# A Strassen-like MLP kernel: C11, C22 and x^T stored ahead of other transfers, and four instruction queues reordered

## What is computed

```python
kv  = einsum('bhsd,bhse->bhde', k, v)            # 8 batches, 8 heads, 576 rows, 64 columns
out = einsum('bhsd,bhde->bhse', q, kv)
x   = out / sqrt(mean(out*out, -1) + 1e-6) * g_norm   # -> 4608 tokens x 512
# first layer (d_ff = 1536)
x = (sigmoid(x @ w_gate) * (x @ w_val)) @ w_out
# second layer
g = x @ w2_gate
out = (g * sigmoid(g) * (x @ w2_val)) @ w2_out    # 4608 x 512, float32
```

## Time and profile before

| | |
|---|---|
| median of three runs | 1748.85 us |
| profiled execution, its own time | 1745.59 us |
| its span (first to last instruction) | 1743.8 us |
| TensorE busy | 1720.7 us, 99% |
| VectorE busy | 1206.9 us, 69% |
| ScalarE busy | 888.8 us, 51% |
| GpSimd busy | 377.8 us, 22% |
| mean granted share of TensorE's clock | 0.997 |
| moved by DMA | 366.93 MB, 210 GB/s |

### The profile page before, as it was taken

One profiled execution on the slowest core, in us unless ns is written; L12 is line 12 of the kernel. 1 busy time (PEld: TensorE's weight loads), 2 busy tenths in 40 slices (PEclk: granted clock), 3 DMA queues, 4 the chain that ended last, 5 costly groups with the idle time before them and its releaser, 6 DMA issues.

```text
span 1743.8 us, 30846 instructions
## 1 busy us (share of the span) xinstructions
PE 1720.7 (99%) x11190; PEld 1689.6 (97%) x11190; DVE 1206.9 (69%) x1938; ACT 888.8 (51%) x1709; POOL 377.8 (22%) x326
## 2 busy tenths in 40 slices
PE   9999999999999999999999999999999999999998
PEld 7899899999999999999998999999999999999998
DVE  4977677787666678666679877787666668655556
ACT  5766566655444445444456555555444445444444
POOL 5722222013111125111136000013111125111111
PEclk9999999999999999999999999999999999999999
DMA  9787786586555576555655555566555567555553
GB/s 243 252 286 196 262 255 200 213 302 224 199 200 199 200 243 228 200 199 200 212 163 215 195 199 200 198 245 240 202 196 202 196 221 239 167 176 190 184 185 92
DMA packets 200151, 366.93 MB, mean 210 GB/s; under 512 B 49984, under 2 KB 160064, under 8 KB 200000
## 3 DMA queue, kind: packets, MB, share of 16 engines
q1 hardware_dynamic: 199776, 364.56, 62.4%
q10 hardware_dynamic: 224, 0.39, 0.1%
HBM read 234.36 MB, written 130.55 MB: 209 GB/s over the span
## 4 chain that ended last, share of the span: by engine, by line
PE 83%; POOL 1%; DVE 1%; DMA 1%; issue 1%; SPq 0%; ACT 0%; DVEq 0%; ACTq 0%; POOLq 0%
PE ps L841 81%; PE ps L764 1%; PE ps L698 0%; DMA wops<-in_q_dram 0%; POOL arena L1659 0%; PE ps L683 0%; DVE arena L1407 0%; DMA xraw<-x 0%; PE ps L688 0%; DVE arena L1389 0%; PE ps L782 0%; PE ps L710 0%; SPq L415 0%; POOL wops L1604 0%; POOL wops L1603 0%
## 5 line engine op out<-in xcount | busy, mean ns | idle before, releaser
L841 PE MATMUL ps<-xo,wa 128*128 128x384 f32 x6048 | 1078.9, 336 | 5.9 <-ACT arena L1038 3.2
L841 PEld LDWEIGHTS ps<-xo,wa 128*128 128x128 f32 x6048 | 1048.6, 188 | 9.6 <-issue 3.6
L1038 ACT ACTIVATE arena<-ps 128x384 f32<-128x384 f32 x648 | 317.1, 491 | 576.9 <-PE ps L841 575.2
L1389 DVE TENSOR_TENSOR arena<-ps,arena 128x384 f32<-128x384 f32 x648 | 352.6, 553 | 362.5 <-PE ps L841 284.3
L841 PE MATMUL ps<-hop,wb 128*128 128x384 f32 x3024 | 538.1, 335 | 1.1 <-DVE arena L1407 0.9
L841 PEld LDWEIGHTS ps<-hop,wb 128*128 128x128 f32 x3024 | 523.0, 188 | 5.0 <-issue 1.7
L1659 POOL TENSOR_TENSOR arena<-arena 128x384 f32<-128x384 f32 x144 | 147.5, 1049 | 734.1 <-DVE arena L1389 734.1
L1339 DVE TENSOR_TENSOR hop<-arena,hop 128x384 fp32r<-128x384 f32 (+1 forms) x396 | 275.9, 719 | 32.8 <-ACT hop L1020 26.8
L1020 ACT ACTIVATE hop<-arena 128x384 fp32r<-128x384 f32 (+1 forms) x396 | 233.4, 609 | 63.6 <-DVE arena L1407 36.0
L1052 ACT ACTIVATE arena<-arena 128x384 f32<-128x384 f32 x216 | 112.7, 522 | 65.2 <-DVE arena L1389 65.1
L1407 DVE TENSOR_TENSOR arena<-arena 128x384 f32<-128x384 f32 x216 | 127.9, 594 | 20.3 <-DVE arena L1389 1.4
(11 more groups left out here) (75 smaller groups left out, 781.9 us busy)
## 6 DMA issues: line engine op xcount, KB each, us to landing
xo<-x_operands SPq DMA_DIRECT2D x168, 768.0 KB, 6.2
x_operands<-xo SPq DMA_DIRECT2D x84, 768.0 KB, 5.3
x<-arena SPq DMA_DIRECT2D x120, 384.0 KB, 3.2
arena<-x SPq DMA_DIRECT2D x96, 384.0 KB, 4.6
xraw<-x SPq DMA_DIRECT2D x22, 768.0 KB, 6.1
wops<-in_moe_w_gate_dram SPq DMA_DIRECT2D x24, 256.0 KB, 4.8
wops<-in_moe_w_val_dram SPq DMA_DIRECT2D x24, 256.0 KB, 4.6
wops<-in_moe_w_out_dram SPq DMA_DIRECT2D x48, 128.0 KB, 2.3
```

The costliest lines, as they stand in the source:

```text
L841: mm = pe.matmul(dst, lhsT, rhs, start=(pr in (1, 5, 2) and c == 0 and i == 0), stop=(c == 1 and i == 2), skip_group_check=(pr in (6, 7, 4 ...
L1038: nc.scalar.activation(dst, X(side), ACT.Copy).then_inc(copied, 1)
L1389: nc.vector.tensor_tensor(dst, acc, buf, ALU.add).then_inc(summed, 1)
```

## The change

Nothing is computed differently, and no instruction of an engine is added or taken away. Instructions move in four queues; TensorE's and GpSimd's own order stay as they are.

- SyncE, at the end of each block: the stores of C11 and C22 go ahead of the third and fourth x operand of the next block. The store of the unit's x^T goes ahead of the stores of C21 and C12. In the blocks of the very first pass the load of the rows of the unit after next also goes ahead of C21 and C12; it stood at the start of the next block.
- ScalarE: in window 1 the copy of a unit's x^T goes ahead of the split of x operand 1 of the next block; in window 2 it goes ahead of the split of operand 7. In a pass's first block the SUMMED split of the fourth set goes behind the copy of product 7, side 0. In block 18 it goes further, behind the copy of side 1.
- VectorE: in block 18 the SUMMED split of set 21 goes behind the hidden values of C11 and C22. In block 17 the two sums that take C21 from its banks (`total_21`) go ahead of the split of operand 5 and of S2.

```diff
@@ sync, start of a block
-                    next_unit(u)
+                    if not (l == 0 and p == 0):
+                        next_unit(u)
@@ sync, end of a block
+                if not last_result(qq):
+                    store_res(qq, 11)
+                    store_res(qq, 22)
                 if prepares and not awaits(nxt, 1):
                     store_xo(nxt, X_ORDER[2])
                     store_xo(nxt, X_ORDER[3])
-                if not last_result(qq):
-                    store_res(qq, 11)
-                    store_res(qq, 22)
+                if is_late(u):
+                    store_xT(u)
+                if prepares and l == 0 and p == 0:
+                    next_unit(u + 2)
                 if not last_result(qq):
                     store_res(qq, 21)
                     store_res(qq, 12)
-                if is_late(u):
-                    store_xT(u)
@@ scalar, s == 5
                             if w == 0 and blk == 0 and qq > 0:
-                                for part in (RAW, SUMMED):
-                                    split_w(6 * (qq // NB) + 3, part)
+                                split_w(6 * (qq // NB) + 3, RAW)
                             if w == 1:
+                                if is_late(u - 1):
+                                    unit_xT(u - 1)
                                 if prepares and not awaits(nxt, 0):
                                     split_x(nxt, 1)
...
-                            if is_late(u - 1):
+                            if w != 1 and is_late(u - 1):
                                 unit_xT(u - 1)
                         if s == 7:
                             copy(7, 0)
+                            if w == 0 and blk == 0 and qq > 0 and qq != LEAP:
+                                split_w(6 * (qq // NB) + 3, SUMMED)
                             if w < 2:
                                 gated(11)
...
                         if s == 9:
                             copy(7, 1)
+                            if w == 0 and qq == LEAP:
+                                split_w(6 * (qq // NB) + 3, SUMMED)
                             if w < 2:
                                 gated(22)
...
                             elif w == 2 and prepares:
                                 split_x(nxt, 6)
-                                split_x(nxt, 7)
                             if is_late(u):
                                 unit_xT(u)
+                            if w == 2 and prepares and not awaits(nxt, 1):
+                                split_x(nxt, 7)
@@ vector, windows 0 and 1
-                        if units and (blk > 0 or w == 0):
+                        if units and (blk > 0 or w == 0 and qq != LEAP):
                             for part in (RAW, SUMMED):
                                 split_w(units[1], part)
...
                         hidden(22)
-                        if units and blk == 0 and w == 1:
+                        if units and blk == 0 and (w == 1 or qq == LEAP):
                             split_w(units[1], SUMMED)
@@ vector, window 2
+                        if p > 0:
+                            total_21(0)
                         if early_x:
                             split_x(nxt, 5)
+                        if is_end(qq, w) or nxt == LEAP:
+                            total_21(1)
+                        if early_x:
                             x_s2(nxt)
-                        if p > 0:
-                            total_21(0)
-                        if is_end(qq, w):
-                            total_21(1)
                         total(12, 0)
```

More of the change, by code:

```diff
@@ L1568, in _ @@
                             x_s1_s3(nxt)
-                        if p > 0 and not is_end(qq, w):
+                        if p > 0 and not is_end(qq, w) and nxt != LEAP:
                             total_21(1)
```

## The result

| | before | after |
|---|---|---|
| median (lowest to highest) of 11 runs each | 1745.69 us (1743.75 to 1754.68) | 1740.35 us (1739.17 to 1741.31) |
| profiled execution, its own time | 1745.59 us | 1741.19 us |
| its span | 1743.8 us | 1738.8 us |

The ratio is 0.9965, with a 95% interval of 0.9953 to 0.9976, so 6.1 us less by the ratio and 5.3 us by the medians. Faster, by less than 0.5%. The forecast was 1742 us, from 6.0 us less.

What follows compares the result with a forecast made beforehand. TensorE was taken as the bound, busy 1720.7 of 1743.8 us, so only 23.1 us of pauses could be won. Units 2.8 plus block 18 3.2 made 6.0 us off 1748.85, 1742.9, forecast as 1742 us, range 1735 to 1750.

Steps and rivals of the forecast that it cites:

- The late units: TensorE's pauses at units in blocks 2 and 3, for x^T copies and late rows: 2.8 us won, bounds 0 and 3.1.
- New waits on DMA at the late units: Sign named for the prediction being wrong: TensorE newly waiting on DMA at the units; the moved load was costed at nothing.
- Block 18: Its entry (0.65 us) and its 3.17 us pause before product 4: 3.2 us won, entry included, taken between 2.5 and 4.6.
- VectorE does the same operations up to the split of operand 6, so all behind keeps its time: Entry of block 18: moving C21's sums forward delays nothing later on VectorE; 0.65 us won.
- The clock: Block 18, after the 3.17 us pause: the lower clock cost 2.8 us; with shorter pauses it stays at its upper level.
- Window 2: Block 18: set 23's load comes no sooner, so TensorE pauses about 1.8 us at the start, behind C21's gate.
- The other first blocks: Blocks 6, 12, 24 and 30, one split moved behind a copy of product 7: 0 us, bounds -0.3 and +0.6.
- All pauses go: Rival, block 18: VectorE's sums come sooner and GpSimd ends early; gain 10.0 us with the units, 1738.9 us; chance 0.13.
- Slower by set 23's weights: Rival, block 18: moved stores delay window 2's weights by 4.4 us; 1.9 us slower in all, 1750.8 us; chance 0.10.
- The units give nothing: Rival: late rows or the x load take over the units' pauses; gain 3.2 us, 1745.7 us; chance 0.12.
- GpSimd hold ScalarE at the split's new place: Rival, block 18: C22's and C21's gates come late, TensorE waits at window 1; gain 2.8 us, 1746 us; chance 0.05.
- The rule's case: Set 23 in block 18, by the VectorE-GpSimd lock alone: 4.6 us there, 7.4 with the units, 1741.5 us; chance 0.15.

Runs made afterwards that it cites:

- e2: Kernel before with only ScalarE's copies of x^T moved ahead of the splits of x operands in windows 1 and 2; 1743.77 us, ratio 0.9981.
- e1: Kernel before with SyncE's reordering alone; 1745.61 us, ratio 0.9996.
- e9: The changed kernel itself, run again on another chip; 1741.29 us, ratio 0.9971.
- e4: Changed kernel with VectorE's order at the end of block 17 put back, split of operand 5 and S2 ahead of C21's sums; 1739.57 us, ratio 0.9959.
- e10: The kernel of e4 run again on another chip; 1740.10 us, ratio 0.9956.
- e8: Changed kernel with GpSimd's six additions in block 17 cut to 8 of 384 columns; run once, 1740.66 us.
- e6: e4 with block 19's x load and set 23's weights sent ahead of operand stores in block 18; 1740.89 us, ratio 0.9962.
- e12: e4 with SUMMED splits behind C21's hidden values (VectorE, windows 0 and 1) or gate (ScalarE, window 1) in all first blocks; 1738.38 us, ratio 0.9950.
- e3: Changed kernel with set 21's SUMMED split put back ahead of both copies of product 7 in block 18; 1741.17 us, ratio 0.9976.

## Why the prediction came out, step by step

**The late units: 2.1 us for 2.8.** The pauses at 179, 191 and 213 are gone as worked out. e2 shows that ScalarE's edit alone removes those at 179 and 213, but then waits of 0.62 and 1.27 us for rows stand at 192 to 195, which SyncE's edit removes. Two points of the step were off. I gave the copies' move 2.5 us and the rows 0.3 us as if they stood apart. By e1 and e2 the copies' move has 1.2 without the rows', and the rows' move has -0.65 without the copies'. And I cost the load's new wait and place at nothing: after, 0.61 us at 268.06 and 0.36 at 138.39 are waits for rows of v that had no such wait before (0.43 and 0.27 in e9). New waits on DMA at the late units were one of the signs that I had named for being wrong.

**Block 18: 2.9 us for 3.2, from pauses partly of other sizes.** The entry at 924.04 (924.05 in the forecast), window 1 with 0.43 us (0.5), window 2 at 956.86 and its side 1 at 958.12 (957.4 and 958.45), and no low clock: these held. The pause of about 1.8 us at the start of window 2 did not come. Up to window 2 TensorE lost 1.2 + 1.4 + 0.7 = 3.4 us from start to start, where I had 0.2 + 1.8 + 0.5 = 2.5, so it came there at about 956.55 and not at 955.7, and waited 0.3 us. Products 7 and 3 together were forecast at 2.0 and took 2.6, and product 7 alone 1.2 for 0.2. The step that failed is "VectorE does the same operations up to the split of operand 6, so all behind keeps its time". The operations are the same, and GpSimd's six additions stand beside them in both kernels, but who comes first has changed. Before, the split of operand 6 started 0.03 us ahead of an addition and took 0.94 us, and the addition took 1.80. After, it starts 0.07 us behind one and takes 1.76. Before:

```profile
925.95 0.94 DVE L1250 TENSOR_TENSOR xo<-xraw,xo 128x768 fp32r<-128x768 f32 x1
925.98 1.80 POOL L1659 TENSOR_TENSOR arena<-arena 128x384 f32<-128x384 f32 x1
...
928.62 0.85 ACT L907 ACTIVATE xo<-xs 128x768 fp32r<-128x768 f32 x1 [0.27 <-DVE xs L1302]
```

After, with the split at 926.10 above:

```profile
926.03 1.02 POOL L1670 TENSOR_TENSOR arena<-arena 128x384 f32<-128x384 f32 x1
...
929.58 0.85 ACT L911 ACTIVATE xo<-xs 128x768 fp32r<-128x768 f32 x1 [1.28 <-DVE xs L1312]
```

In the same way the split of operand 5 took 1.42 us for 0.94. S2 was shorter, 1.30 for 1.77. It ended at 925.19 rather than 924.17 because the two sums of C21 stand ahead of it. The seven operations that end with the split of operand 6 (two splits, S2 and four sums) take 6.2 us, where they took 5.3. So the operand sum behind them (L1312) and ScalarE's split of it come 0.96 us later, and ScalarE's copy of product 6, with two splits of weights between, 0.95 us later. e4 and e10 show the size of it: without the edit the entry costs 0.61 us and product 7 nothing; with it the entry costs nothing, product 7 takes 1.05, and window 1 is reached 0.6 us later. In e8, with the additions cut, the splits of operands 5 and 6 took 0.94 and 0.96 us and the pause at product 7 is gone.

**The clock: right in direction, not a fixed price.** The 2.8 us rested on one profile. e1 and e2 had the same pause, and by their frames, 1.2 us shorter, the clock took about 1.6 us. The gain of the change in block 18 was therefore 2.9 us against the profile shown, and 1.7 to 2.0 us against the kernels e1 and e2.

**Window 2.** I took 3.2 between the bounds 2.5 and 4.6, and 2.88 was measured. GpSimd's four steps ended at 954.56, 0.65 us sooner, with a last step of 0.73 us for 1.42. ScalarE's SUMMED split and the gate of C21 behind it, which stood at 957.04 and 958.72, came at 954.59 and 956.29. Set 23's load did not come sooner, as forecast. e6 shows that a sooner load alone does not help.

**The other first blocks: 0 in the forecast, a gain of 0 to 0.15 us each measured.** That is within the scatter: e9 has 32.48 to 32.57 us, the kernel before 32.46 to 32.61.

**Stores in the second layer: forecast 0, measured 0.94 us.** This was outside the argument. In block 23 the next pass's first weights, set 24, now land sooner behind stores that have left. GpSimd starts on them at 1159.21, 12.7 us into the frame; before it was 1164.07, 14.8 us into it. Before, GpSimd's sums ran beside VectorE's splits of hidden values (L1339), two of which took 2.10 us:

```profile
1164.07 0.74 POOL L1601 TENSOR_TENSOR wops<-wops 128x256 f32<-128x256 f32 x1 [208.86 <-DMA wops<-in_moe_w_gate_dram]
...
1169.90 2.10 DVE L1339 TENSOR_TENSOR hop<-arena,hop 128x384 fp32r<-128x384 f32 x2
...
1180.26 2.03 PE L841 MATMUL ps<-hop,wb 128*128 128x384 f32 x10 [0.47 <-DVE arena L1407]
```

The same three after, where the same two splits (L1349) took 1.01 us and TensorE didn't wait:

```profile
1159.21 0.74 POOL L1612 TENSOR_TENSOR wops<-wops 128x256 f32<-128x256 f32 x1 [204.65 <-DMA wops<-in_moe_w_gate_dram]
...
1166.61 1.01 DVE L1349 TENSOR_TENSOR hop<-arena,hop 128x384 fp32r<-128x384 f32 x2
...
1176.11 3.12 PE L845 MATMUL ps<-hop,wb 128*128 128x384 f32 x17
```

The frame is 31.73 to 31.76 us in every kernel with SyncE's edit, e1 among them. In e2, without it, it is 32.09, as GpSimd happened to start sooner than in the profile of before. So 0.35 to 0.94 us belong to the stores.

**What was luck.** The sum of 6.0 us is near the measured 5.3 to 6.1, but the two terms that I had gave 2.08 + 2.88 = 4.96. The rest is the stores' 0.94, which I had not seen, and 0.2 that is scatter. And 1742 us was taken from a first median of 1748.85, which is 3.2 us above the later one of eleven runs.

**The rivals.** "All pauses go" did not come: `total(11, 0)` is late by VectorE's own queue, and even e8 keeps the pauses at window 1 and 2. "Slower by set 23's weights" did not come, as set 23 landed 0.3 us later and not 4.4. "The units give nothing" did not come either: they gave 2.08 us. Nor did GpSimd hold ScalarE at the split's new place: it was done with set 21 at 936.06, and ScalarE started the split at 938.45. The rule's case took it that all four of GpSimd's steps shorten to 0.74 us. At set 23 they took 0.74, 1.34, 1.46 and 0.73, where they had taken 0.74, 1.33, 1.72 and 1.42: only the last became short.

The rule is that of the Trainium skill (SBUF — State Buffer, "Who interferes with whom"): a VectorE instruction with both inputs in SBUF and a GpSimd instruction that reads SBUF keep each other out for a whole instruction. The trace agrees, at 0.96 us for the split of operand 6 with GpSimd's additions cut (e8) and 1.76 behind one of them. I had used it at set 23 and not at the entry, where the edit itself moved VectorE's work against GpSimd's.

**Open.** Why the clock was low for 6.83 us in one execution and 3.41 in two others behind an equal pause was not tried. How much of e12's 2.9 us beyond some 1.5 us is its order is open too. No run has SyncE's move in block 17 or in block 23 alone.

## To carry to other kernels

When operations of VectorE with two inputs in SBUF are reordered, price them anew by what GpSimd does at their new time: here a split took 0.94 us when it started just ahead of an addition and 1.76 just behind one. Two edits that remove one long pause don't add: measure each with the other undone, on frames cut at the same matmuls of both kernels, since scatter elsewhere (2.3 us here) is as large as the effect. A wait taken from TensorE needs its successor fed too: copies without rows gave 1.2 us, rows without copies no gain, both 2.1, each give or take the scatter of 1.1 us.

## What the runs showed of the hardware that was not expected

- One 128x768 fp32 operation of VectorE took 0.94 to 0.96 us with GpSimd's additions of 128x384 cut or when it started just ahead of one, and 1.30 to 1.77 behind one. A 128x384 split took 0.5 us, and 1.05 beside GpSimd's sums of weights. Six additions cut to 8 of 384 columns (e8) took 3.0 us off TensorE's way to window 1.
- Behind pauses of 3.17 to 3.19 us the granted clock was at its lower level for 6.83 us once and 3.41 us twice. Behind all shorter pauses of the MLPs, the longest of 1.63 us (e3), it stayed up.
- The clock was low in the attention at the start in six of the fourteen profiled executions: for 3.41 us in four, 6.83 in e8 and 23.9 in e4, where TensorE was busy all of 23.00 us. That execution's time was 1747.95 us, where the other five runs of e4 had a highest of 1741.87.
